# Attention and a ReLU-squared feed-forward on one core: the first transfer through two queues, and eleven warm-up multiplications for thirteen

## The reference

```
scores = q @ k^T / sqrt(64)
scores = cap * tanh(scores / cap)
attn   = exp(scores - max(scores))
attn   = attn / (sum(attn) + 1e-9)
x      = (attn @ v), heads side by side, 1792 tokens x 768
h      = x @ w_in
g      = s * relu(h)^2 + b
out    = g @ w_out
```

## Time and profile before

| | |
|---|---|
| median of 3 runs | 593.14 us (592.75 to 593.47) |
| profiled execution, its own time | 593.31 us |
| its span, first to last instruction | 591.5 us |
| PE busy | 585.2 us, 99% |
| DVE busy | 424.6 us, 72% |
| ACT busy | 341.0 us, 58% |
| POOL busy | 183.1 us, 31% |
| packets of the one hardware queue | 61568, 118.09 MB |

### The profile page before, as it was taken

How to read it: one execution, slowest core, us unless ns; L and a number is a source line. 1 busy time by engine, 2 the same in 40 slices (tenths; PEclk the granted TensorE clock), 3 DMA queues, 4 the chain that set the end, 5 groups by cost and what they waited for, 6 DMA issues and landing times.

```text
span 591.5 us, 8822 instructions
## 1 busy us (share of the span) xinstructions
PE 585.2 (99%) x3074; PEld 469.1 (79%) x3074; DVE 424.6 (72%) x645; ACT 341.0 (58%) x406; POOL 183.1 (31%) x143
## 2 busy tenths in 40 slices
PE   8999999999999999999999999999999999999997
PEld 4335777768878777777777999999999999999997
DVE  4987899978668768769774125568878998775453
ACT  7985775775675666666652455546456445543330
POOL 0013966503434344434324333141333332100000
PEclk9999999999999999999999999999999999999999
DMA  8422445343555545555544878978676899854532
GB/s 282 169 94 93 121 146 167 114 126 152 203 188 197 199 149 192 197 207 185 215 143 155 323 256 289 325 249 279 231 273 229 291 308 318 288 172 125 172 110 92
DMA packets 61611, 118.65 MB, mean 201 GB/s; under 512 B 6464, under 2 KB 44160, under 8 KB 61568
## 3 DMA queue, kind: packets, MB, share of 16 engines
q1 hardware_dynamic: 61568, 118.09, 58.1%
HBM read 78.75 MB, written 39.32 MB: 200 GB/s over the span
## 4 chain that ended last, share of the span: by engine, by line
PE 95%; ACT 2%; DVE 1%; issue 1%; DVEq 0%; ACTq 0%
PE banks L758 14%; PE banks L760 13%; PE banks L759 13%; PE banks L798 12%; PE banks L797 12%; PE banks L796 12%; PE banks L703 9%; PE banks L659 5%; PE banks L605 2%; PE banks L725 2%; PE banks L683 1%; ACT e L957 1%; ACT e L907 1%; PE banks L816 1%; PE banks L736 0%
## 5 line engine op out<-in xcount | busy, mean ns | idle before, releaser
L758 PE MATMUL banks<-x_hi,w_hi 128*128 128x448 f32 x384 | 142.7, 372 | 0.0
L760 PE MATMUL banks<-x_hi,w_lo 128*128 128x448 f32 x384 | 140.4, 366 | 0.0
L759 PE MATMUL banks<-x_lo,w_hi 128*128 128x448 f32 x384 | 140.3, 365 | 0.0
L797 PE MATMUL banks<-x_lo,w_hi 128*128 128x448 f32 x336 | 122.8, 365 | 0.0
L796 PE MATMUL banks<-x_hi,w_hi 128*128 128x448 f32 x336 | 122.7, 365 | 0.0
L798 PE MATMUL banks<-x_hi,w_lo 128*128 128x448 f32 x336 | 122.7, 365 | 0.0
L964 ACT ACTIVATE hidden_sb<-banks 128x448 f32<-128x448 f32 x56 | 30.5, 545 | 100.4 <-PE banks L760 100.4
L758 PEld LDWEIGHTS banks<-x_hi,w_hi 128*128 128x128 f32 x384 | 72.1, 188 | 20.3 <-issue 14.0
L982 ACT ACTIVATE x_hi<-e,beside 128x448 fp32r<-128x448 f32 x64 | 48.8, 763 | 49.9 <-PE banks L798 49.9
L957 ACT ACTIVATE e<-e,beside 128x1792 f32<-128x1792 f32 (+1 forms) x48 | 76.2, 1607 | 1.2
L760 PEld LDWEIGHTS banks<-x_hi,w_lo 128*128 128x128 f32 x384 | 72.1, 188 | 5.9
(11 more groups left out here) (129 smaller groups left out, 797.3 us busy)
## 6 DMA issues: line engine op xcount, KB each, us to landing
t_scratch<-work SPq DMA_DIRECT2D x32, 448.0 KB, 3.2
e<-t_scratch SPq DMA_DIRECT2D x64, 224.0 KB, 4.2
hidden_scratch<-hidden_sb SPq DMA_DIRECT2D x56, 224.0 KB, 1.9
work<-hidden_scratch SPq DMA_DIRECT2D x24, 448.0 KB, 4.1
e<-hidden_scratch SPq DMA_DIRECT2D x48, 224.0 KB, 3.8
beside<-q_k SPq DMA_DIRECT2D x23, 448.0 KB, 4.8
work<-w_out SPq DMA_DIRECT2D x16, 384.0 KB, 3.6
s_scratch<-work SPq DMA_DIRECT2D x16, 384.0 KB, 2.9
```

The lines of the kernel that those rows point to most:

```text
L758: nc.tensor.matmul(out, w_hi[:, j, w], x_hi[:, batch % 2, c, :], start=c == 0, stop=False)
L759: nc.tensor.matmul(out, w_hi[:, j, w], x_lo[:, batch % 2, c, :], start=False, stop=False)
L760: last = nc.tensor.matmul(out, w_lo[:, j, w], x_hi[:, batch % 2, c, :], start=False, stop=c == CT - 1)
L797: nc.tensor.matmul(out, w_tile(w_hi_flat, i, k, d), ring(x_lo, n), start=False, stop=False)
```

## The change

The first transfer is split in two by partitions: SyncE issues rows 0 to 63, ScalarE rows 64 to 127, as the first instruction of its program. Each adds 16 to `lead_in`, so both waits now ask for 32. The multiplications of ones ahead of the first scores are eleven and not thirteen.

```diff
-WARM_UP = 13
+WARM_UP = 11
@@ sync
-            sp.dma_start(beside[:, 0:LEAD], lead[:, 0:LEAD]).then_inc(lead_in, 16)
+            sp.dma_start(beside[0:D, 0:LEAD], lead[0:D, 0:LEAD]).then_inc(lead_in, 16)
@@ tensor, first_scores
-                    pe.wait_ge(lead_in, 16)
+                    pe.wait_ge(lead_in, 32)
@@ scalar, ahead of its first wait
+            act.dma_start(beside[D:P, 0:LEAD], lead[D:P, 0:LEAD]).then_inc(lead_in, 16)
+
             act.wait_ge(ones_ready, 1)
@@ vector
-            dve.wait_ge(lead_in, 16)
+            dve.wait_ge(lead_in, 32)
```

## The result

| | before | changed |
|---|---|---|
| median, 16 runs each | 593.22 us (592.75 to 593.62) | 594.39 us (593.95 to 595.12) |
| ratio | | 1.0022, 95% interval 1.0016 to 1.0029 |
| profiled execution, its own time | 593.31 us | 594.03 us |
| its span | 591.5 us | 592.2 us |

The changed kernel is 1.17 us slower in the median. The prediction, 593.0 in a range of 592.3 to 594.2, missed the sign and, by 0.2 us, the range. The profiled execution of the changed kernel is one of its faster ones: it shows 0.72 of the 1.17 us.

What follows compares the result with a forecast made beforehand. PE, busy 99% of the span, was taken to hand any start gain to the end; the smaller of 0.20 (clock) and 0.11 us (DVE's slack), so 0.1 us, gave 593.2 profiled, 593.0 in the median's terms, range 592.3 to 594.2.

Steps and rivals of the forecast that it cites:

- Bounds, handing on: PE over the whole execution: busy 99% of the span, so what the start loses or wins reaches the end one for one.
- Part 1: PE's warm-ups at the start: two fewer save 0.43 us, so PE is free for the first score at 3.52.
- Part 2: Landing of the lead, the first transfer: last half at 3.5, unchanged; first score at 3.55, 0.40 us sooner.
- late bound: Last half's landing if both queues are served by turns: one issue of 0.39 to 0.62 us later, 3.9 to 4.1.
- Part 3: ACT and SP at the start: ACT's extra issue costs nothing; SP's queue 0.2 us sooner to 0.4 later.
- Part 4: From first scores to 23.77: clock rise unmoved at about 6.3, so 0.20 of 0.40 us is kept; DVE cuts it to 0.1.
- Rival B: PE idles before the late half, the clock rises later, slow passes cost 0.37 us more each: 593.6, chance 0.12.
- DVE's leg: DVE's work behind w_in piece 0 (8.30), up to 16.82: only 0.11 us of slack, so the gain is 0.1 us.
- Rival C: ACT's half of the lead issued behind its table load, landing at 4.8, first score 0.9 us late: 594.2, chance 0.15.
- mild form: Milder case of Rival C, shared issue hardware: lead lands 3.9 to 4.1, 0 to 0.2 us later; no separate chance.

Runs made afterwards that it cites:

- e1: Kernel before with only the warm-ups changed, 11 for 13, the lead one whole transfer on SyncE's queue: 592.90 us against 593.10, ratio 1.0000.
- f4: The same kernel as e1 run again, 11 warm-ups alone against the kernel before: 593.16 us beside 593.14, ratio 1.0000.
- f1: The changed kernel run once more, nothing altered, against the kernel before: 594.22 us, ratio 1.0017.
- e3: Changed kernel with both 64-row halves on SyncE's queue, one behind the other, 11 warm-ups: 594.18 us, ratio 1.0020 to the kernel before.
- f3: Changed kernel with the halves cut by columns (128 rows of 1168 bytes each), two queues, 11 warm-ups: 593.01 us, ratio 1.0000 to the kernel before.
- f2: Changed kernel with 15 warm-ups for 11 and nothing else: 593.34 us, ratio 1.0003 to the kernel before.
- e2: Changed kernel with 13 warm-ups again, so only the split by partitions differs from the kernel before: 593.46 us, ratio 1.0011.
- e5: Kernel before with 5 warm-ups for 13, transfers as before: 593.50 us, ratio 1.0008.
- e7: Kernel before with 20 warm-ups for 13, transfers as before: 594.15 us, ratio 1.0019.
- e4: Kernel before with 11 warm-ups, lead whole on SyncE's queue and the second transfer on ScalarE's, issued at once: 594.08 us, ratio 1.0019.

## Why the prediction was wrong

**Bounds, handing on.** Right. What is lost at L925 reaches the end one for one, shown by the constant 583.7 in twelve of the thirteen executions.

**Part 1**, eleven warm-ups free PE at 3.52: right, as far as e1 and f4 can show (first score 3.61 and 3.77, both waiting for the lead, holes of 0.20 and 0.36). That this is worth little: right.

**Part 2, the landing, is the first step that failed.** "I take 3.5, no change, the nearest row being the whole transfer itself." It was 4.10 in the profile after, 4.17 in f1, at or just past the late bound of 3.9 to 4.1. The row that stood nearer in form, the 64-row transfer of 0.62 us, was used for the late bound alone: a 64-row issue takes 0.55 to 0.58 us, and two of them side by side end little sooner than two in a row (e3). The Trainium skill's sentence in "DMA: Bandwidth & Descriptors", section "Issuing engines are not separate DMA queues", that several engines save only the time to initiate the DMA, agrees with e3 and f3: at best 0.17 us saved by the second queue in the one, none in the other that can be told from f4.

**Part 3.** ACT's table load did come behind its DMA (1.32), and nothing on ACT or DVE was late by it. SP's queue ran 0.6 us late (its first w_in issue at 2.70 for 2.12), more than the 0.4 allowed. Right as to cost.

**Part 4, the clock, is the second step that failed, and the larger.** "If the rise comes at the same time" was the condition. Before, the turn was between 5.60 and 6.33; it was past 7.34 in the changed kernel and past 9.02 in f1. What it costs is the difference f1 - f2, 0.88 us, of a loss of 1.08 (594.22 - 593.14); the rest, 0.20 (f2) to 0.36 (e2; 0.65 by its ratio), is the late lead with PE kept busy or nearly so. The Trainium skill, "TensorE: Matmul & The Clock Gate", section "What's actually happening", has the rise go by time and not by a number of matmuls. That agrees with e1 and f4 (turn near 5.3 and before 4.61, with two warm-ups fewer than before). But these two executions of one program also show that no one time can be carried from one profile to another, and in the changed kernel the rise did not keep its time. Rival B had this mechanism at 0.12 and 593.6; it priced the passes rightly (0.37 us more each), and came out 0.8 us below the measured time because it kept the 0.20 us won and left out the late lead.

**DVE's leg.** It was taken to cap the gain. In the changed kernel w_in's first piece came at 7.66 and not at 8.30, and ACT alone set L1064 (17.60). In e1, f3 and f4 it was at 8.07, 7.84 and 7.43: the piece's landing moves by more than the slack of 0.11 us that the sum rested on. So that cap of 0.1 us was a reading of one execution.

**Rival C** had the sign and nearly the size (594.2), by another way, so that this was luck: the half was not queued behind the table load but went out at 0.73. Its deciding point, a landing past 3.9, was right. Its mild form, "landing 3.9 to 4.1, 0 to 0.2 us later", was what came, and was under-priced because it left the clock out: the late lead and the hole were treated as two rivals, and are one.

**Still open:** what in a hole decides the rise. e5's is twice as long and earlier, and did not hold the turn beyond 6.64; e2's 0.44 did not either; 0.71 to 0.89 us up to 4.1 or later did in all four profiles that had it. And why the form of 64 rows takes its queue longer, and its last packet is followed so late by the engine that waits; the runs show only that it is so.

## What to carry to other kernels

Filler work ahead of the first real multiplication is sized against the landing of the data it waits for: too much costs most of what it lasts (e7), too little cost nothing measurable with holes of 0.20 to 0.36 us before data that came by 3.8 us (e1, f3, f4), but a hole of 0.78 us before a late first transfer cost some 0.9 us through slower multiplications behind it (f1 against f2). The length of the hole alone is no measure: one of 1.49 us that ended at 3.62 cost 0.41 us, not clear of nothing (e5). So a change that may make the first transfer late must not take away cover in the same edit; measure the landing first. If a transfer must be cut, the cut by columns was free here and the cut by partitions was not, and a second queue did not bring the bytes in sooner.

## What the runs showed of the hardware

- A 64-row transfer of 2336 bytes a row keeps its queue 0.55 to 0.58 us, on SyncE and on ScalarE, alone or beside another; 128 rows of 2336 or of 1168 bytes keep it 0.38 to 0.41 us. The next transfer in SyncE's queue, 128 rows of 1280 bytes, keeps it 0.42 us behind a whole lead and 0.57 to 0.82 us behind a 64-row half (0.82 in the changed kernel, 0.57 in f2, 0.58 in e3).
- Two 128-row transfers issued together on two queues (292 and 160 KB) are issued in 0.39 and 0.41 us, but the first lands 0.4 to 0.6 us later than alone (DVE's start 4.11 against 3.52 to 3.75 in before, e1 and f4), its last packet ending at 3.67 against 3.16 to 3.33.
- Two 64-row halves on two queues end their last packet at 3.32 (changed kernel), no later than the whole lead in f4 (3.33), and yet DVE starts at 4.10 and not at 3.75.
- The rise of TensorE's clock came before 4.61 us in one of the thirteen profiles and after 9.02 in another, and more than half a microsecond apart in two executions of one program (e1 and f4). Executions of one kernel spread by 0.5 (e4, f1) to 1.5 us (e2) in time. In the two programs with two profiles the start of L925 accounts for 0.32 of 0.41 us (e1, f4) and 0.47 of 0.51 us (changed, f1).
